# Slots directly behind the members, turned rows one gather at a time, and result rows a whole bank at a time

## What is computed

```python
def _moe_ref(x, w_gate, w1, w2):
    N, D = x.shape            # 1536, 512
    E = w_gate.shape[1]       # 8
    cap = N // E              # 192
    logits = x @ w_gate
    flat = logits.flatten()
    order = np.argsort(-flat)
    for idx in order:         # greedy: best pair (token, expert) first
        tok, e = (int(idx) // E, int(idx) % E)
        if assigned[tok] >= 0 or counts[e] >= cap:
            continue
        assigned[tok] = e
        counts[e] += 1
    for e in range(E):
        mask = assigned == e
        h = np.maximum(x[mask] @ w1[e], 0.0)   # 512 -> 1024
        out[mask] = h @ w2[e]                  # 1024 -> 512
```

## Time and profile before

| | |
|---|---|
| device time, median of 3 runs | 642.2 us (641.81 to 643.93) |
| profiled execution | 641.11 us, of which the span is 639.1 us |
| PE busy | 619.7 us (97%) |
| PEld busy | 482.4 us (75%) |
| DVE busy | 360.8 us (56%) |
| ACT busy | 295.3 us (46%) |
| POOL busy | 146.8 us (23%) |
| chain that ended last | PE 91%, DVE 4%, ACT 1%, issue 1%, DMA 1% |
| attention, first layer, second layer (us from the start) | 0 to 255, 255 to 508, 508 to 639 |

### The profile page before, as it was taken

How to read it: one execution, slowest core, us unless ns; L and a number is a source line. 1 busy time by engine, 2 the same in 40 slices (tenths; PEclk the granted TensorE clock), 3 DMA queues, 4 the chain that set the end, 5 groups by cost and what they waited for, 6 DMA issues and landing times.

```text
span 639.1 us, 11496 instructions
## 1 busy us (share of the span) xinstructions
PE 619.7 (97%) x4384; PEld 482.4 (75%) x4384; DVE 360.8 (56%) x1132; ACT 295.3 (46%) x539; POOL 146.8 (23%) x152
## 2 busy tenths in 40 slices
PE   6999999999999999888999999999999999999996
PEld 3767777777767766367898989898899877777773
DVE  6876777677776776886968778786512220000000
ACT  5877777777777676542525344352212111111111
POOL 5340303031322921210110101010342124333201
PEclk9999999999999999999999999999999999999999
DMA  8938836455454100272644435373897769999970
GB/s 184 240 87 187 191 80 157 99 136 125 109 186 97 51 11 1 108 278 70 222 143 147 157 132 196 118 257 110 278 358 275 271 217 326 341 367 350 333 268 20
DMA packets 73393, 116.38 MB, mean 182 GB/s; under 512 B 33799, under 2 KB 37161, under 8 KB 73058
## 3 DMA queue, kind: packets, MB, share of 16 engines
q1 hardware_dynamic: 68738, 106.75, 54.1%
q0 software_dynamic: 4016, 8.80, 4.0%
q10 hardware_dynamic: 576, 0.01, 0.0%
HBM read 87.76 MB, written 12.23 MB: 156 GB/s over the span
## 4 chain that ended last, share of the span: by engine, by line
PE 91%; DVE 4%; ACT 1%; issue 1%; DMA 1%; SPq 0%; POOL 0%; POOLq 0%; DVEq 0%
PE psB L1061 14%; PE psB L1075 13%; PE psB L353 10%; PE psB L338 9%; PE psB L1804 9%; PE psB L1819 9%; PE psA L323 7%; PE psA L325 5%; PE psB L368 2%; PE psA L997 2%; PE psB L1096 1%; PE psB L281 1%; PE psB L292 1%; PE psA L1036 1%; PE psB L1989 1%
## 5 line engine op out<-in xcount | busy, mean ns | idle before, releaser
L474 DVE TENSOR_REDUCE mx<-psA 128x1 f32<-128x768 f32 x96 | 91.8, 956 | 52.1 <-PE psA L325 50.6
L542 ACT ACTIVATE prob<-psA,ebi,esc 128x768 f32<-128x768 f32 x96 | 95.2, 992 | 23.8 <-DVE ebi L419 19.4
L1061 PE MATMUL psB<-xgT,w 128*128 128x192 f32 x512 | 91.4, 331 | 0.3 <-ACT xgT L1159 0.3
L1075 PE MATMUL psB<-hT,w 128*128 128x192 f32 x512 | 88.2, 329 | 0.0
L1061 PEld LDWEIGHTS psB<-xgT,w 128*128 128x128 f32 x512 | 82.5, 190 | 6.6 <-issue 5.9
L1075 PEld LDWEIGHTS psB<-hT,w 128*128 128x128 f32 x512 | 82.7, 190 | 0.3
L338 PE MATMUL psB<-cst,prob 128*128 128x128 f32 x576 | 78.8, 273 | 0.3
L323 PE MATMUL psA<-kH,qT 128*128 128x384 f32 x192 | 74.2, 387 | 2.8 <-ACT kB L581 1.6
L338 PEld LDWEIGHTS psB<-cst,prob 128*128 128x128 f32 x576 | 66.8, 140 | 5.3 <-DVE pT L487 1.9
L353 PE MATMUL psB<-pT,v_in 128*64 128x384 f32 x360 | 68.0, 499 | 0.0
L593 ACT COPY pT<-psB 128x512 f32<-128x512 f32 x96 | 55.9, 582 | 25.6 <-PE psB L338 25.0
(11 more groups left out here) (289 smaller groups left out, 877.8 us busy)
## 6 DMA issues: line engine op xcount, KB each, us to landing
w<-in_moe_w SPq DMA_DIRECT2D x34, 2048.0 KB
kH<-hi SPq DMA_DIRECT2D x30, 192.0 KB
q_in<-in_q SPq DMA_DIRECT2D x16, 192.0 KB, 4.1
k_in<-in_k SPq DMA_DIRECT2D x16, 192.0 KB, 4.3
v_in<-in_v SPq DMA_DIRECT2D x8, 384.0 KB, 3.6
x_scratch<-x_of_batch SPq DMA_DIRECT2D x2, 1536.0 KB, 6.8
x_scratch<-x SPq DMA_DIRECT2D x8, 384.0 KB
qT<-hi SPq DMA_DIRECT2D x15, 192.0 KB
```

The costliest lines, as they stand in the source:

```text
L474: nc.vector.tensor_reduce(mx[:, u:u + 1], psS[u % 2][:, :, 0:HALF], AX.XY, ALU.max).then_inc(s_dv, 1)
L542: nc.scalar.activation(prob[:, u % 2, :, :], psS[u % 2][:, :, 0:HALF], ACT.Exp, bias=ebi[:, u:u + 1], scale=esc[:, u:u + 1], accum_out=den ...
L1061: ins = nc.tensor.matmul(ps[:, (f % 2) * CAP:(f % 2 + 1) * CAP], w1[:, k % 2, d, f * P:(f + 1) * P], xgT[:, k % 2, d, :], start=d == 0, st ...
L1075: ins = nc.tensor.matmul(ps[:, (d % 2) * CAP:(d % 2 + 1) * CAP], w2[:, k % 2, f, d * P:(d + 1) * P], hT[:, k % 2, f, :], start=f == 0, sto ...
```

## The change

- `slots` is called directly behind `members` on DVE: its twelve comparisons come before the update of `M` (`full`, `M`, `m`), no longer after it. `tokens` and two small updates (`left`, `open_`, now a function `gone`) follow after `m`.
- On PE the step "tokens" comes before "best". In rounds 2 to 6 nothing stands between the two. In round 1, warm matmuls stand there: 7, places, 3, tokens, 6, best, 14 (before: 7, places, best, 3, tokens, 20).
- A step `xt` turns one gather (96 rows, all four column pieces) and waits for that gather alone. The first `h` waits for the copy of the second.
- `rw` is two steps of four transposes in place of four of two, each copied by ACT as 96x512 in place of 96x256 twice. An expert then has 22 steps and takes 12 uses of banks, before 24 and 14. The last expert keeps its four short ones. The numbers in `some` are lowered by the steps that are gone, so that the other steps stand where they stood.
- "ranks" begins with the four tiles that DVE copies and ends with the eight that ACT copies.

```diff
-        rw = [("rw", k - 1, i, a) for i in range(2) for a in range(2)]
-        return q + rw[:2] + [("lt", k - 1)] + h[:4] + [("lx", k - 1)] + rw[2:] + h[4:] + y
+        rw = [("rw", k - 1, i, 2) for i in range(2)]
+        return q + rw[:1] + [("lt", k - 1)] + h[:4] + [("lx", k - 1)] + rw[1:] + h[4:] + y
...
-        some = [1, 0, 0, 8, 2, 5, 3, 1, 1, 1, 2] if r > 1 else [1, 1, 0, 4, 0, 3, 2, 1, 1, 0, 1]
+        some = [1, 0, 0, 8, 1, 5, 2, 1, 1, 1, 2] if r > 1 else [1, 0, 0, 4, 0, 3, 2, 1, 1, 0, 1]
         if r:
             idle(r - 1, 7)
             steps.append(("places", r - 1))
             fill(some[0])
+            idle(r - 1, 3)
+            steps.append(("tokens", r - 1))
+            idle(r - 1, 20 if r > 1 else 6)
+            steps.append(("best", r))
+            idle(r - 1, 14)
+            work += expert(r - 1)
         else:
             idle(r, 4)
-        steps.append(("best", r))
-        fill(some[1])
+            steps.append(("best", r))
         if r:
-            idle(r - 1, 3)
-            steps.append(("tokens", r - 1))
-            idle(r - 1, 20)
-            work += expert(r - 1)
+            fill(some[1])
...
-                for j in range(NJ):
+                for j in list(range(8, NJ)) + list(range(8)):
...
-                if half == 0:
-                    for n in (2 * k, 2 * k + 1):
-                        pe.wait_ge(s_xg[n % NX], 16 * (n // NX + 1))
-                for c in range(2):
-                    for i in range(2):
-                        ins = nc.tensor.transpose(
-                            ps[:, c * CAP + i * HT:c * CAP + (i + 1) * HT],
-                            xg[0:HT, (2 * k + i) % NX, (2 * half + c) * P:(2 * half + c + 1) * P],
-                            cst[0:HT, C_ID:C_ID + HT])
+                pe.wait_ge(s_xg[n % NX], 16 * (n // NX + 1))
+                for c in range(KD):
+                    ins = nc.tensor.transpose(ps[:, c * HT:(c + 1) * HT], xg[0:HT, n % NX, c * P:(c + 1) * P],
+                                              cst[0:HT, C_ID:C_ID + HT])
...
-                    if f == 0 and d % 2 == 0:
-                        pe.wait_ge(s_e, emptied(("xt", k, d // 2)))
+                    if f == 0 and d == 0:
+                        pe.wait_ge(s_e, emptied(("xt", k, 1)))
...
+                pieces = range(KD) if a == 2 else range(2 * a, 2 * a + 2)
+                pe.wait_ge(s_e, emptied(("y", k, pieces[-1] // 2)))
...
             elif st[0] == "best":
                 r = st[1]
+                slots(dve, r - 1)
+                link(dve, nc.vector.tensor_scalar(full[:, :], cnt[:, :], float(CAP), -BIG, ALU.is_ge, ALU.mult))
+                link(dve, nc.vector.tensor_tensor(M[:, :, :], M[:, :, :], full[:, :].unsqueeze(1).to_broadcast(allj),
+                                                  ALU.add))
                 nc.vector.tensor_reduce(m[:, :], M[:, :, :], AX.X, ALU.max).then_inc(s_m, 1)
+                tokens(dve, r - 1)
+                gone(dve, r - 1)
                 dve.wait_ge(s_m, r)
-                slots(dve, r - 1)
-                tokens(dve, r - 1)
                 pick(nc, dve, link, M[:, :, :], tie, m[:, :], wk[:, :, :], top[:, :],
                      Ob[:, r % 2, :, 0:E], known=True).then_inc(s_O, 1)
```

More of the change, by code:

```diff
@@ L745, in middle_plan @@
         todo = expert(k)
-        todo.insert(14, ("place", 2 * k - 2, 2))
+        todo.insert(12, ("place", 2 * k - 2, 2))
         if k == NEARLY + 1:
-            todo.insert(6, ("place", 0, 2 * NEARLY))
+            todo.insert(5, ("place", 0, 2 * NEARLY))
         steps += todo
@@ L946, in rows_out @@
     def rows_out(k):
-        return emptied(("rw", k, 1, 1))
+        return emptied(("rw", k, 1, 1 if k == E - 1 else 2))
     def enter(pe, n):
@@ L1014, in tensor @@
                     ins = nc.tensor.matmul(psC[:, j * E:(j + 1) * E], cT[:, j * P:(j + 1) * P], selE[:, :],
-                                           start=j == 0, stop=j == NJ - 1, skip_group_check=True)
+                                           start=j == 8, stop=j == 7, skip_group_check=True)
                 ins.then_inc(s_rk, 1)
@@ L1039, in tensor @@
             elif st[0] == "xt":
-                _, k, half = st
+                _, k, i = st
+                n = 2 * k + i
                 ps = enter(pe, use[st])
-                if half == 0:
-                    for n in (2 * k, 2 * k + 1):
-                        pe.wait_ge(s_xg[n % NX], 16 * (n // NX + 1))
-                for c in range(2):
-                    for i in range(2):
-                        ins = nc.tensor.transpose(
-                            ps[:, c * CAP + i * HT:c * CAP + (i + 1) * HT],
-                            xg[0:HT, (2 * k + i) % NX, (2 * half + c) * P:(2 * half + c + 1) * P],
-                            cst[0:HT, C_ID:C_ID + HT])
+                pe.wait_ge(s_xg[n % NX], 16 * (n // NX + 1))
+                for c in range(KD):
+                    ins = nc.tensor.transpose(ps[:, c * HT:(c + 1) * HT], xg[0:HT, n % NX, c * P:(c + 1) * P],
+                                              cst[0:HT, C_ID:C_ID + HT])
                 ins.then_inc(s_f, 1)
@@ L1093, in tensor @@
                 ps = enter(pe, use[st])
[L1094 to L1097, removed]
+                pieces = range(KD) if a == 2 else range(2 * a, 2 * a + 2)
+                pe.wait_ge(s_e, emptied(("y", k, pieces[-1] // 2)))
+                for c in pieces:
+                    ins = nc.tensor.transpose(ps[0:HT, (c - pieces[0]) * P:(c - pieces[0] + 1) * P],
+                                              yT[:, k % 2, c, i * HT:(i + 1) * HT], cst[:, C_ID:C_ID + P])
                 ins.then_inc(s_f, 1)
@@ L1155, in scalar @@
             elif st[0] == "xt":
-                _, k, half = st
+                _, k, i = st
                 n = use[st]
                 act.wait_ge(s_f, n + 1)
-                nc.scalar.copy(xgT[:, k % 2, 2 * half:2 * half + 2, :],
-                               psW[n % NWB][:, 0:2 * CAP].rearrange("p (c t) -> p c t", c=2)).then_inc(s_e, 1)
+                nc.scalar.copy(xgT[:, k % 2, :, i * HT:(i + 1) * HT],
+                               psW[n % NWB][:, 0:KD * HT].rearrange("p (c t) -> p c t", c=KD)).then_inc(s_e, 1)
             elif st[0] == "h" and st[2] % 2:
@@ L1177, in scalar @@
                 act.wait_ge(s_f, n + 1)
-                nc.scalar.copy(x1[:, 2 * k + i, 256 * a:256 * a + 256], psW[n % NWB][0:HT, 0:256]).then_inc(s_e, 1)
+                cols = slice(0, DM) if a == 2 else slice(256 * a, 256 * a + 256)
+                nc.scalar.copy(x1[:, 2 * k + i, cols], psW[n % NWB][0:HT, 0:cols.stop - cols.start]).then_inc(s_e, 1)
             elif st[0] == "lt":
@@ L1224, in slots, with gone @@
         ins.then_inc(s_sl, 1)
+    def gone(dve, k):
         if k < ROUNDS:
@@ L1325, in vector @@
                     members(dve, r)
-                    link(dve, nc.vector.tensor_scalar(full[:, :], cnt[:, :], float(CAP), -BIG, ALU.is_ge, ALU.mult))
-                    link(dve, nc.vector.tensor_tensor(M[:, :, :], M[:, :, :], full[:, :].unsqueeze(1).to_broadcast(allj),
-                                                      ALU.add))
             elif st[0] == "places" and st[1] >= ROUNDS - 1:
@@ L1331, in vector @@
                 slots(dve, st[1])
+                gone(dve, st[1])
                 tokens(dve, st[1])
```

## The result

The changed kernel took 649.03 us (median of 6, 646.68 to 651.29) against 643.07 for the kernel before on the same chip (median of 6, 641.80 to 644.32): a ratio of 1.0103 (95% interval 1.0081 to 1.0124). A second series of runs gave 1.0093 (1.0070 to 1.0115). The ratio is not the quotient of the two medians, so the two ways of counting differ by some tenths of a microsecond. It is slower, as forecast, but by 6.0 us between the medians, and by 6.6 us by the ratio, where I had 4.2. The profiled execution took 646.68 us, its span is 644.7 us.

What follows compares the result with a forecast made beforehand. In rounds 2 to 6 of the first layer PE was taken as the bound. The terms +5.2, +0.9, -0.3 and -1.6 sum to +4.2 us, on 642.2 giving 646.4 us; range 643.6 to 649.2.

Steps and rivals of the forecast that it cites:

- The ends of rounds 2 to 5: First layer, four round ends: row transposes no longer cover the comparisons, PE's y work starts 1.3 us later each, +5.2 us.
- The end of round 1: Once: slots and tokens start 0.45 us earlier, but 1.31 us of transposes come behind the tokens, +0.9 us.
- Whole banks: Row transposes of the experts: fewer waits for a bank, 0.2 us each for seven experts plus 0.2, -1.6 us.
- One of the signs that I named: At the row transposes of results: L1096 would show no wait on ACT.
- The end of round 0: Once: slots and gathers 0.46 us earlier, best later, first h slightly earlier; -0.3 us in all (-0.6 to +0.4).
- the order of "ranks": Round 0, where nothing covers it: starting "ranks" on DVE's tiles gains 0.1 us.
- The rival of the clock: Round ends: granted clock falls to the lower level, five y steps take up to twice 6.6 us, 680 us; chance 0.03.

Runs made afterwards that it cites:

- only PE's order changed: Changed kernel with 11 warm matmuls for 3 between places and tokens of round 0, and VectorE's order put back: 646.20 us, ratio 1.0067 to the kernel before.
- two y steps: Changed kernel with two y steps in place of one between places and tokens in rounds 2 to 6, one fewer behind: 640.67 us, ratio 0.9991.
- banks alone: Changed kernel with the order at the end of a round put back as in the kernel before: 641.30 us, ratio 0.9991.
- both waits filled: Changed kernel with 11 warm matmuls (round 0) and two y steps (rounds 2 to 6) before tokens: 639.60 us, 0.9961; with six warm matmuls moved behind best, 639.07, 0.9947.
- VectorE's order alone: Changed kernel with 11 warm matmuls for 3 between places and tokens of round 0, and PE's order put back: 651.72 us, ratio 1.0158 to the kernel before.

## Why the prediction was right or wrong

**The ends of rounds 2 to 5** (+5.2 in the sum, 1.3 each): right. The order costs 1.30 us an end, 30.08 against 28.78 over three rounds, and for the reason given: PE waits for the hits behind one y step, and VectorE's slots start no earlier, since PE's positions set them. The kernel with only PE's order changed shows that it is PE's, and the one with two y steps that the wait is all of it.

**The end of round 1** (+0.9): right; +0.96 stands in the table, with the banks' part in it. The slots started 0.46 us earlier against the first h, as forecast (0.45), and PE waited 1.20 us for the hits.

**Whole banks** (-1.6): the size was a little off. I had 0.2 for each expert; 0.13 a round was measured. The rest of the layer, where nothing of the order changes, gave 0.91 in the table, more than the 0.6 that I had for it. Together in this profile: 5 x 0.13 + 0.91 = 1.6. The medians can't confirm it: the kernel with banks alone is 0.1% faster, and its interval reaches past no change. One of the signs that I named did not come: the row transposes of results (L1098, before L1096) still found PEld idle for ACT, 2.1 us in five times and 0.9 in six, where it had been 2.1, 1.3 and once 0.4. So most of these waits stayed. Where h's relu had held rw in expert 6, the transposes now follow one another (0.22 of lx and 0.44 of rw in the place of a wait for ACT and 0.42).

**The end of round 0** (-0.3): this is the step that failed. The part that I worked out was right: with a full clock the first h comes 24.35 or 24.39 us behind the first best, before 24.81, so -0.4. (The 0.1 in it for the order of "ranks" was not measured by itself.) What I left out was the stand, and what it does to the clock, which stood in no term of the sum. I wrote that the tokens start at 272.56 and that PE then goes on, and costed six warm matmuls at 1.3 from a row at full clock. But the same shift puts only three warm matmuls (0.6 us) into the 2.5 us of the slots and comparisons in which the kernel before had 1.3 us of transposes as well. PE stood 1.95 us, the clock fell, and the stretch cost +1.05 in place of -0.3 or -0.4. That is the missing 1.4 us of the profile: 4.2 + 1.4 = 5.6, which is what the spans differ by. (The other stretches of the table are off from their terms by up to 0.4 us each way, and these cancel.) In the medians it is 1.0093 or 1.0103 against 1.0062 with that wait filled, some 2 to 2.6 us.

**The rival of the clock.** I gave it 0.03, and with another place: the ends of rounds 2 to 5, at 6.6 us each. There it never came, with waits of 1.2 us. It came where PE has filler only, in round 0, where I had looked at the row of 5 us with 3.55 busy and concluded that gaps of this size don't matter. The longest wait of PE in that row is 0.95 us, so it couldn't speak for one of 1.95. The Trainium skill, "TensorE: Matmul & The Clock Gate", section "HAM oscillation — how this bites in real kernels", tells of waits between bursts of matmuls that bring PE back to half its clock. The trace agrees in kind (clock 0.64 and 0.50 behind the stand of round 0), though the waits of that section are longer ones, for transfers; here 1.95 us was enough in four of five profiles. I should have set the warning against each stand that the change makes, the one of round 0 too.

**The medians.** With the stand of round 0 filled the loss is 4.0 us by the ratio (1.0062), close to the 4.2 that I had forecast, without a fall. The changed kernel's executions reach from 646.6 to 651.4, those of before from 640.3 to 644.3, those with that stand filled from 645.1 to 646.4, and those with both waits filled (two kernels) from 638.9 to 642.2. Where the clock falls in the slowest of the changed kernel (mean clock 0.990, where the profiled ones have 0.997) no profile shows; that part is open.

## What to carry to other kernels

When one engine's long piece (here 2.25 us of comparisons) hides beside another's work, write down what covers it before moving either: moving the 1.31 us of transposes behind it cost 1.30 us at each of four ends, and moving one more step of work in front gave all of it back. Starting a step earlier on its own engine is worth nothing where the engine that uses its result stands in order behind another wait. And after a change, look for each place where TensorE now stands in one piece, not only at the waits' sum: eight more matmuls on constants in round 0 were worth 0.3 to 0.4% here, in two pairs of kernels (1.0093 and 1.0103 to 1.0062, and 0.9991 to 0.9961).

## What the runs showed of the hardware

The granted clock fell to the lower level behind a stand of 1.95 us, for some 3 to 4 us, in four of five profiles of the same schedule, and stayed full in the fifth; in the other program, with a stand of 1.87 or 1.88 us, it fell in one of two. Waits of 1.2 us (and of 1.9, in one kernel) between the long runs of matmuls of rounds 2 to 5 left it full in every profile. And it fell once behind two waits of 0.67 and 0.66 us at the first xt and h (VectorE's order alone), where the same two waits (0.66 and 0.66) left it full with banks alone. So the length of the last stand by itself doesn't tell whether the clock falls, and one profile doesn't either.

What a fall costs depends on what stands behind it: in the changed kernel the slow matmuls lay in front of the transposes on which the rest waited, for 1.2 to 1.5 us; in the kernel before without ten warm matmuls they lay beside the wait for a gather, for 0.1 us. The second thing is that a gather early in the second layer landed 2 to 3 us late in two profiles of one kernel, and the clock fell behind that wait too (0.66, and 0.82 and 0.76).
